# A three-stage recurrent mixer on one NeuronCore: theta's low part moved to VectorE, the token weights' low parts moved in GpSimd's order, wider attention pieces, and one mixing unit issued in two parts

## What is computed

```
for t in range(S):                              # stage 1, a linear recurrence
    state = alpha[t][:, None] * state + outer(k[t], v[t])
    y[t] = q[t] @ state
x = y, heads side by side                       # (batch, 768, 384)
theta = x @ w_theta                             # stage 2
zr, zi = x * cos(theta), x * sin(theta)
u = x + w_tok_r @ zr + w_tok_i @ zi             # mixes positions
x2 = u + relu(u @ w_ch)
h = relu(x2 @ w_in); u, v = halves of h         # stage 3
out = (u * (w_spatial @ layernorm(v) + b)) @ w_out
```

## Time and profile before

| | |
|---|---|
| median of 3 runs | 583.96 us (583.91 to 584.16) |
| the profiled execution, its own time | 582.94 us |
| span of its profile | 581.2 us |
| PE busy | 565.3 us (97%), 5982 matmuls and as many loads |
| DVE busy | 397.0 us (68%) |
| ACT busy | 246.8 us (42%) |
| POOL busy | 231.5 us (40%) |
| chain that ended last | PE 79%, DVE 10%, ACT 4%, POOL 2%, issue 2%, DMA 2% |

### The profile page before, as it was taken

How to read it: one execution, slowest core, us unless ns; L and a number is a source line. 1 busy time by engine, 2 the same in 40 slices (tenths; PEclk the granted TensorE clock), 3 DMA queues, 4 the chain that set the end, 5 groups by cost and what they waited for, 6 DMA issues and landing times.

```text
span 581.2 us, 14059 instructions
## 1 busy us (share of the span) xinstructions
PE 565.3 (97%) x5982; PEld 537.6 (93%) x5982; DVE 397.0 (68%) x625; ACT 246.8 (42%) x461; POOL 231.5 (40%) x185
## 2 busy tenths in 40 slices
PE   6889999999999999999999999999999999999997
PEld 5678899999999999999999989999999899989997
DVE  7888998787776876776544279977537752776253
ACT  3757655453544544544453135822432243134210
POOL 2756343442332522422413047363813471347131
PEclk9989999999999999999999999999999999999999
DMA  8942322221322332323033180200220022002002
GB/s 314 341 164 79 120 79 71 96 86 69 111 69 70 111 110 93 115 71 111 2 111 122 42 285 1 82 0 1 83 81 2 0 82 82 0 2 83 0 1 81
DMA packets 21230, 49.71 MB, mean 86 GB/s; under 512 B 1712, under 2 KB 16816, under 8 KB 20656
## 3 DMA queue, kind: packets, MB, share of 16 engines
q1 hardware_dynamic: 21168, 48.81, 24.4%
HBM read 39.37 MB, written 9.44 MB: 84 GB/s over the span
## 4 chain that ended last, share of the span: by engine, by line
PE 79%; DVE 10%; ACT 4%; POOL 2%; issue 2%; DMA 2%; SPq 0%; DVEq 0%; ACTq 0%
PE psY L532 18%; PE psC L564 6%; PE psC L488 5%; PE psY L709 4%; PE psY L660 4%; PE psY L670 3%; PE psF L650 3%; PE psS L709 3%; PE psF L709 3%; PE psS L429 3%; PE psY L650 2%; PE psS L660 2%; PE psS L670 2%; PE psF L670 2%; PE psC L709 2%
## 5 line engine op out<-in xcount | busy, mean ns | idle before, releaser
L1374 POOL TENSOR_TENSOR z_lo<-cos_sin,z_hi 128x768 fp32r<-128x768 f32 x23 | 43.9, 1911 | 87.5 <-ACT z_hi L827 87.5
L1451 POOL TENSOR_TENSOR gated_lo<-raw_gated,gated_hi 128x384 fp32r<-128x384 f32 x32 | 36.0, 1130 | 70.3 <-ACT gated_hi L976 69.1
L1361 POOL TENSOR_TENSOR akq<-akq 128x512 f32<-128x512 f32 x23 | 27.4, 1192 | 66.9 <-DVE akq L1043 66.9
L1381 POOL TENSOR_TENSOR u_lo<-u_f,u_hi 128x384 fp32r<-128x384 f32 x24 | 29.2, 1247 | 48.3 <-ACT u_hi L832 48.3
L532 PE MATMUL psY<-tok_r_hi,z_hi 128*128 128x384 f32 x123 | 43.2, 351 | 0.7 <-POOL z_lo L1374 0.6
L532 PE MATMUL psY<-tok_i_hi,z_lo 128*128 128x384 f32 x123 | 41.2, 335 | 0.0
L532 PE MATMUL psY<-tok_r_hi,z_lo 128*128 128x384 f32 x123 | 41.2, 335 | 0.0
L532 PE MATMUL psY<-tok_i_lo,z_hi 128*128 128x384 f32 x123 | 41.2, 335 | 0.0
L532 PE MATMUL psY<-tok_r_lo,z_hi 128*128 128x384 f32 x123 | 41.1, 334 | 0.0
L532 PE MATMUL psY<-tok_i_hi,z_hi 128*128 128x384 f32 x123 | 41.1, 334 | 0.0
L976 ACT ACTIVATE gated_hi<-raw_gated 128x384 fp32r<-128x384 f32 x32 | 16.4, 527 | 58.0 <-DVE raw_gated L1283 57.3
(11 more groups left out here) (309 smaller groups left out, 1818.9 us busy)
## 6 DMA issues: line engine op xcount, KB each, us to landing
akq<-akq SPq DMA_DIRECT2D x22, 770.0 KB, 5.0
v<-v_in SPq DMA_DIRECT2D x24, 192.0 KB, 5.2
x_dram<-u_f SPq DMA_DIRECT2D x8, 576.0 KB, 3.6
out<-ot SPq DMA_DIRECT2D x24, 192.0 KB, 1.9
raw_x<-x_dram SPq DMA_DIRECT2D x3, 1152.0 KB, 5.1
raw_tok_r<-w_tok_rT SPq DMA_DIRECT2D x6, 384.0 KB, 6.7
raw_tok_i<-w_tok_iT SPq DMA_DIRECT2D x6, 384.0 KB, 8.1
raw_sp<-w_spT SPq DMA_DIRECT2D x4, 576.0 KB, 6.0
```

The costliest lines, as they stand in the source:

```text
L1374: pool.tensor_tensor(Z[c][1][:], trigs[g % 2][:], f(Z[c][0][:]), ALU.subtract).then_inc(z_lo, 1)
L1451: pool.tensor_tensor(GA[1][:, j, half(h)], ug[:, j, half(h)], f(GA[0][:, j, half(h)]), ALU.subtract).then_inc(g_lo, 1)
```

## The change

It does four things.
- Chunks 0, 1 and 2 use two pieces of 64 columns in `keys_values` and `attend` where all chunks used four of 32.
- Theta's low part is made on VectorE, between `update_state(1)` and `multiply_z(0)`, and no longer on GpSimd.
- GpSimd makes `tok_low(0)` in its place. `tok_low(1)` to `tok_low(4)` each move one wait for `multiply_z` later, and `tok_low(5)` stands behind `z_low(3)`.
- Unit `yb` of every chunk with c = 0 goes through `first_mix`, its high parts first, then its low part. Before, only that of chunk 6 did. The waits of `first_mix` count z over the batches.

```diff
-QUARTERS = tuple(slice(32 * i, 32 * i + 32) for i in range(4))
+IN_HALVES = 3
+PIECES = [tuple(slice(w * i, w * i + w) for i in range(P // w)) for w in (64, 32)]
...
                 for p in range(PAIRS):
-                    for q, rows in enumerate(QUARTERS):
+                    for rows in PIECES[g >= IN_HALVES]:
+                        h = rows.start // 64
                         mm = pe.matmul(psK[rows, HD * p:HD * (p + 1)], kT[:, p, rows],
-                                       V[g % 2][:, HD * (2 * p + q // 2):HD * (2 * p + q // 2 + 1)], start=True, stop=True)
+                                       V[g % 2][:, HD * (2 * p + h):HD * (2 * p + h + 1)], start=True, stop=True)
...
-                        for rows in QUARTERS:
+                        for rows in PIECES[g >= IN_HALVES]:
...
                 if parts == Z_HIGH:
                     pe.wait_ge(tok_lo, s // 2 * 2 + 2)
-                    pe.wait_ge(z_hi, s + 1)
+                    pe.wait_ge(z_hi, k // HALVES * CHUNKS + s + 1)
                 else:
-                    pe.wait_ge(z_lo, s + 1)
+                    pe.wait_ge(z_lo, k // HALVES * CHUNKS + s + 1)
...
-                        if g == CHUNKS:
+                        if c == 0:
                             first_mix(yb, range(CT), Z_HIGH)
                             first_mix(yb, range(CT), Z_LOW)
...
                 update_state(c)
+                if c == 1:
+                    dve.wait_ge(theta_hi, 1)
+                    dve.wait_ge(theta_made, 1)
+                    dve.tensor_tensor(WT[1][:], raw_theta[:], f(WT[0][:]), ALU.subtract).then_inc(theta_lo, 1)
                 multiply_z(c - 1)
...
             scale_queries(2)
-            pool.wait_ge(theta_hi, 1)
-            pool.wait_ge(theta_made, 1)
-            pool.tensor_tensor(WT[1][:], raw_theta[:], f(WT[0][:]), ALU.subtract).then_inc(theta_lo, 1)
             tok_low(0)
-            tok_low(1)
             for c in range(2, CHUNKS):
                 pool.wait_ge(z_mul, c - 1)
-                tok_low(c)
+                tok_low(c - 1)
                 if c < CHUNKS - 1:
                     scale_queries(c + 1)
                     z_low(c - 2)
             z_low(CHUNKS - 3)
+            tok_low(CHUNKS - 1)
             scale_queries(CHUNKS)
```

## The result

| | before | changed |
|---|---|---|
| median, measured side by side on one chip (6 runs each) | 583.42 us (582.75 to 584.16) | 580.85 us (579.99 to 582.49) |
| the profiled execution, its own time | 582.94 us | 581.29 us |
| span of its profile | 581.2 us | 579.5 us |
| PE busy | 565.3 us, 5982 matmuls | 566.0 us (98%), 5806 matmuls |
| POOL busy | 231.5 us | 226.5 us |

The ratio is 0.9961 [0.9949, 0.9974]: **2.3 us faster** (1.5 to 3.0), where the forecast was 1.4. The direction was right and the size 0.9 us too small. The lines of the changed kernel stand two to seven further down: the queries are scaled in L1368, the token parts made in L1375 and z's low part in L1381 on GpSimd; VectorE's scans are L1027 and L1046, the keys L1035, `multiply_z` L1090, theta's low part L1152; the scores are L431.

What follows compares the result with a forecast made beforehand. PE bounds the kernel behind 75 us, VectorE sets the pace in the first batch. +0.6 - 2.7 + 1.2 - 0.5 = -1.4 us from the 583.96 median gives 582.6 us; own range 581.9 to 583.2, with rivals 1 and 2 581.0 to 584.1.

Steps and rivals of the forecast that it cites:

- rival 2: End of batch 0: tok_low(5) costs nothing because L1032 starts first, the 1.2 us stays; 581.4 us, chance 0.12.
- Theta's part: VectorE's gap before multiply_z(0): theta's low part is held 0.2 to 0.3 us, multiply_z(0) starts 0.6 us late.
- The token parts: First batch, multiply_z(0) to multiply_z(1): L1032 and L1043 no longer blocked, period 9.32 in place of 12.01, 2.7 us less.
- tok_low(5): End of batch 0: behind z_low(3) on GpSimd it holds VectorE's L1032; 1.2 us given back, bounds nothing and 1.8.
- rival 1: Stretch from 58 to 65 us: one more VectorE instruction collides with GpSimd, another 1.2 us goes; 583.8 us, chance 0.22.
- One sign that I had named for being wrong: PE between 55 and 75 us: a new wait there would show the prediction wrong.
- The half pieces: keys_values and attend, chunks 0 to 2: 128 instructions halved, counted as nothing; lower bound 1.0 us less PE a chunk.
- The signs that I had named for being wrong: Chunks 0 to 2: L440, L454 and L463 taking longer than 0.55, 0.86 and 0.88 would show the prediction wrong.
- Rival 3: keys_values and attend, chunks 0 to 2: half pieces run one by one, 8.2 us more in all; 587.9 us, chance 0.08.
- The two-part unit: Last unit, chunks 12 and 18: 0.5 us each on the spot, chunk 18's turning into a longer wait; 0.5 us gained.

Runs made afterwards that it cites:

- The two undone halves: Two edits of the changed kernel: theta's low part back on GpSimd (ratio 0.9975); old order of the token parts with theta on VectorE (ratio 0.9977).
- late parts again: Unaltered second measurement of the changed kernel in which VectorE makes token part 5 and GpSimd part 7 behind z_low(4); 579.88 us, ratio 0.9933.
- the fourth experiment: Late token parts exchanged in the changed kernel: VectorE makes part 5 in place of part 7, GpSimd part 7 behind z_low(4); 579.67 us, ratio 0.9939.

## Why the prediction was right, and where it was too small

The mechanism was right in its main terms, and the size was too small. By the time alone one would have chosen the wrong cause: 583.96 us times 0.9961 is 581.7 us, just under the 581.9 to 583.2 that the forecast gave itself and nearest to the 581.4 of rival 2, whose cause the traces rule out.

**Theta's part: right.** It started in the gap, was held 0.22 us, and `multiply_z(0)` came 0.52 us later against its own `update_state(1)`; 0.6 was forecast.

**The token parts: right.** The period fell from 12.01 to 9.30 us, forecast 9.32, because both blocked instructions became free. The two undone halves show the split: 1.4 us for the order, 0.8 us for theta. They also show that they need each other: theta on VectorE without the new order puts a token part in front of `multiply_z(0)` and is worse at that point than the kernel before (13.98 us from `update_state(1)` to `multiply_z(1)`, against 13.26).

**tok_low(5): right.** 1.85 us for L1035 where 1.9 was forecast, 1.13 us given back where 1.2 was. Rival 2, that it might cost nothing, fell, and rival 1, another collision, did not come. One sign that I had named for being wrong did come, a new wait of PE between 55 and 75 us:

```profile
61.45 0.45 PE L491 MATMUL psC<-theta_hi,xT_hi 128*128 128x384 f32 x1 [0.59 <-DVE xT_lo L1073]
```

It is no cost of its own but the way in which the 1.2 us reach PE: it is gone where the exchange takes them away. The exchange of the late parts shows the cause, since the 1.2 us vanish with it.

**The half pieces: right in sum, wrong in size.** "I take nothing, because quarter pieces do run side by side." The sum needed no more, since the cost is hidden, but PE's work grew by 0.37 us in a chunk rather than staying or shrinking. The signs that I had named for being wrong came: the groups took up to 0.67 and 1.12 us, where 0.55 and 0.88 were the limit (L457 took 0.85 to 0.87, with 0.86 as its limit). Rival 3, one piece at a time, would have been 2.9 us a chunk and is far off. Whether something comes back from the smaller count of instructions early on is open.

**The two-part unit: this is the term that was mis-sized.** At 0.5 us for each place it was right (0.58 measured at chunk 12, 0.57 by the kernel with the unit whole). What failed is the step behind it: "Those hang on a load, two scans and GpSimd's low parts of u, none of which moves: there the gain turns into a longer wait." I had read the load's landing time, 6.2 us, off one profile as if it belonged to the kernel. It does not. The same load, in twelve of its readings, all that had a wait for the queries among them:

| kernel, chunk | landed after | wait for the queries |
|---|---|---|
| after, 14 and 20 | 4.5, 4.7 us | none |
| changed kernel again, 14 and 20 | 4.8, at most 4.2 us | none |
| before, 14 and 20 | 5.3, 6.2 us | none, 0.32 us |
| only the wide pieces on before, 20 | at most 4.2 us | none |
| four pieces, 20 | 5.9 us | 0.53 us |
| late parts changed over, 14 | 5.9 us | 0.50 us |
| late parts again, 14 | 5.5 us | 0.15 us |
| decays loaded behind v, 14 and 20 | 6.5, 5.9 us | 0.87, 0.80 us |

So chunk 20 gave 0.99 us where I had 0. From chunk 19's scores to chunk 20's it took 14.24 us before and 13.24 after; with a whole unit and no wait for queries it took 13.84 (and 13.84 at chunk 14 of the kernel before). That makes 0.6 us of the unit and 0.4 of a wait that a fast load takes away in any kernel: the kernel before with the wide pieces alone had a fast one and no wait, and the changed kernel with four pieces had a slow one and waited. So the new program does not make the load fast. Only the first is the change's, and it is kept in most executions: of the eighteen readings of two-part kernels with the load in its usual place three had a wait, 0.15 to 0.53 us. With 0.5 at both places the forecast would have been -1.9 us, inside the measured 1.5 to 3.0.

**A term that the prediction did not have** is the 0.35 us ahead of chunk 12, which goes with theta's instruction and whose cause stays open. With what the steps measured, the change's own sum is +0.52 - 2.71 + 1.13 - 0.35 - 0.58 - 0.6 = -2.6 us. The rests differ by 3.1: the 0.4 us of the load comes on top, and 0.1 us is not assigned.

**The start-up was in neither the sum nor a rival.** It is 1.4 us, and it hides nearly half of the gain when one profile of each is compared: 582.94 and 581.29 us differ by 1.65, the rests by 3.1. The 2.3 us of all runs lie between, and the two groups of runs, compared each with its like, give 2.5 to 2.9, near the sum's 2.6. The median of 583.96 us from which the forecast started came from three runs that all lie in the upper group.

## What to carry to other kernels

When VectorE and GpSimd both subtract tiles of SBUF, write down for each which one starts first and when the other's next two-tile instruction comes: moving a GpSimd instruction behind a VectorE one that it blocked gives back what that one lost (here 1.5 us for the keys and 1.4 for the scan), and the instruction moved out of one place must be followed to the next place where it blocks. A gain that leads to a wait on a load is neither lost nor kept: read the landing time in several executions before giving it zero. Before comparing one profile with another, look where in the groups of runs each lies. Fewer and wider TensorE instructions were no saving here, where the narrow ones already run side by side.

## What the runs showed of the hardware

- **Two start-ups.** The first 16 score matmuls, at 7.8 to 8.3 us, took 2.08 us in seven of the fourteen profiles and 1.16 to 1.50 in the others, also for the same kernel. The ten matmuls behind them went the same way, 2.15 us in the changed kernel and 1.31 in the fourth experiment. `update_state(1)` came at 21.86 to 22.30 us in the first kind and at 20.42 to 20.60 in the second. The granted clock of 8 to 12 us reads 1.00 in both kinds, so the rows do not show what slowed the matmuls.
- **Landing times.** In its usual place the 770 KB load of chunks 14 and 20 landed after 4.2 us or less to 6.2 us, while the DMA engines moved about 85 GB/s in that stretch; the same program read 5.9 and 5.5 us at chunk 14 in two executions. With two-part units PE did not wait up to 5.1 us, and waited from 5.5 us on; with the whole unit it did not wait at 5.3 us.
- **Column pieces.** 64 matmuls of 32 columns took 0.80 us to the next group and 32 of 64 columns 1.01 us; for the 96-wide ones the two are nearly alike (0.66 and 0.68).
- **A wait that lowers the clock.** In a wait of 3.06 us the granted clock fell to 0.50, and it read 0.50 for the 4 us from 24 us on, in the kernel with the old order. The usual wait at that place, 1.44 or 1.45 us, went either way: the clock stayed at 1.00 in the changed kernel and read 0.57 for those 4 us in the kernel with the whole unit, where `multiply_z(1)` then came 9.70 us behind `multiply_z(0)` and not 9.30. So the length of the one wait does not decide it.
